# Moving the feed-forward weight loads to ScalarE's DMA queue, splitting the tile-load wait by tensor, and dropping the filler matmuls of the first three tiles

## What is computed

```python
# recurrence, per batch and head, over t
m_new = maximum(f_t + m, i_t)
C = exp(f_t + m - m_new) * C + exp(i_t - m_new) * outer(v_t, k_t)
n = exp(f_t + m - m_new) * n + exp(i_t - m_new) * k_t
y_t = sigmoid(o_t) * (C @ q_t) / maximum(abs(n . q_t), 1)
# x: (3072, 320) = y as tokens
g = maximum(x @ w_in, 0) ** 2          # w_in 320 x 2048
x2 = g @ w_out                         # w_out 2048 x 320
e = argmax(x2 @ w_gate); p = softmax(x2 @ w_gate)[e]
out = p * (maximum(x2 @ w1[e], 0) @ w2[e])   # 8 experts, 1024 wide
```

## Time and profile before

| what | before |
|---|---|
| median of three runs | 846.07 us (844.88 to 847.69) |
| the profiled execution, its own time | 849.91 us |
| its span | 848.0 us |
| PE busy | 798.2 us (94%) |
| DVE busy | 565.3 us (67%) |
| POOL busy | 378.6 us (45%) |
| ACT busy | 243.4 us (29%) |

### The profile page before, as it was taken

One profiled execution on the slowest core, in us unless ns is written; L12 is line 12 of the kernel. 1 busy time (PEld: TensorE's weight loads), 2 busy tenths in 40 slices (PEclk: granted clock), 3 DMA queues, 4 the chain that ended last, 5 costly groups with the idle time before them and its releaser, 6 DMA issues.

```text
span 848.0 us, 17409 instructions
## 1 busy us (share of the span) xinstructions
PE 798.2 (94%) x5334; PEld 759.0 (90%) x5335; DVE 565.3 (67%) x1075; ACT 243.4 (29%) x578; POOL 378.6 (45%) x346
## 2 busy tenths in 40 slices
PE   7769899999999999999999999988879999999994
PEld 7769899999999999999999999987769988898984
DVE  5758886667666767766766767465846657766662
ACT  2114334333333333333334333334000112021320
POOL 3326654533533533433434432777200263438792
PEclk9759899999999999999999999999989999999997
DMA  9955333233331442331432300545421061616640
GB/s 182 188 120 127 65 55 59 57 57 57 84 58 21 99 65 43 81 64 29 100 62 40 82 1 4 191 144 165 138 65 37 19 198 31 182 28 187 187 142 23
DMA packets 153815, 74.98 MB, mean 88 GB/s; under 512 B 107951, under 2 KB 147887, under 8 KB 153744
## 3 DMA queue, kind: packets, MB, share of 16 engines
q1 hardware_dynamic: 141552, 48.07, 27.6%
q10 hardware_dynamic: 9120, 17.30, 7.0%
q0 software_dynamic: 3072, 8.68, 2.7%
HBM read 62.89 MB, written 12.39 MB: 89 GB/s over the span
## 4 chain that ended last, share of the span: by engine, by line
PE 61%; issue 18%; POOL 7%; DVE 4%; POOLq 3%; ACT 2%; DMA 2%; SPq 2%; DVEq 0%; ACTq 0%
PE bank_h L1213 20%; PE bank_o L1377 18%; POOL expert_w L547 5%; PE bank_b L1275 5%; PE bank_o L1457 2%; PE bank_c L1280 2%; PE bank_c L1267 2%; PE bank_a L1286 2%; PE bank_h L1432 1%; PE bank_h L1359 1%; PE bank_a L1255 1%; POOLq L630 1%; PE bank_b L1255 1%; DVE decay L967 1%; PE bank_c L1294 1%
## 5 line engine op out<-in xcount | busy, mean ns | idle before, releaser
L598 POOL TENSOR_TENSOR g_lo<-g,g_hi 128x384 fp32r<-128x384 f32 x128 | 138.5, 1083 | 241.3 <-ACT g_hi L678 240.7
L547 POOL TENSOR_TENSOR expert_w<-raw,expert_w 128x1024 fp32r<-128x1024 f32 (+2 forms) x48 | 105.4, 2222 | 95.3 <-ACT expert_w L649 93.5
L678 ACT CAST g_hi<-g 128x384 fp32r<-128x384 f32 x128 | 66.0, 516 | 270.9 <-DVE g L838 262.9
L1377 PE MATMUL bank_o<-wout_hi,g_hi 128*128 128x320 f32 x384 | 129.9, 338 | 6.4 <-POOL g_lo L598 6.1
L1377 PE MATMUL bank_o<-wout_hi,g_lo 128*128 128x320 f32 x384 | 120.3, 313 | 0.0
L1377 PE MATMUL bank_o<-wout_lo,g_hi 128*128 128x320 f32 x384 | 120.1, 313 | 0.0
L1457 PE MATMUL bank_o<-expert_w,hT_hi 128*128 (+1 forms) x448 | 103.9, 320 | 6.8 <-DVE hT_lo L1156 4.5
L838 DVE TENSOR_TENSOR g<-relu 128x384 f32<-128x384 f32 x128 | 82.1, 642 | 33.8 <-ACT relu L738 19.7
L649 ACT CAST expert_w<-raw 128x1024 fp32r<-128x1024 f32 (+2 forms) x48 | 44.0, 981 | 197.1 <-PE bank_h L1436 126.3
L1377 PEld LDWEIGHTS bank_o<-wout_hi,g_hi 128*128 128x128 f32 x384 | 73.5, 191 | 11.1 <-POOL g_lo L598 7.9
L1457 PEld LDWEIGHTS bank_o<-expert_w,hT_hi 128*128 128x128 f32 x448 | 76.2, 193 | 7.9 <-issue 7.9
(11 more groups left out here) (261 smaller groups left out, 1632.4 us busy)
## 6 DMA issues: line engine op xcount, KB each, us to landing
forget_bc<-forget_rows SPq DMA_DIRECT2D x48, 256.0 KB, 4.5
raw<-in_moe_w_dram ACTq DMA_DIRECT2D x12, 512.0 KB, 3.6
raw<-in_moe_w_dram ACTq DMA_DIRECT2D x12, 480.0 KB
ex_x<-regions SPq DMA_DIRECT2D x28, 192.0 KB
q_in<-in_q_dram SPq DMA_DIRECT2D x24, 160.0 KB, 3.2
k_in<-in_k_dram SPq DMA_DIRECT2D x24, 160.0 KB, 3.9
v_in<-in_v_dram SPq DMA_DIRECT2D x24, 160.0 KB, 4.3
o_in<-in_o_gate_dram SPq DMA_DIRECT2D x24, 160.0 KB, 4.2
```

Of the source, the lines that this page charges most:

```text
L547: pool.tensor_tensor(lo, raw[0:rows, slot, 0:cols], hi[0:rows].bitcast(F32), ALU.subtract).then_inc(lo_split, 1)
L598: pool.tensor_tensor(g_lo[:, r, :], g[:, s, :], g_hi[:, r, :].bitcast(F32), ALU.subtract).then_inc(glo_ready, 1)
L678: act.copy(g_hi[:, r, :], g[:, s, :]).then_inc(ghi_ready, 1)
L1377: ins = pe.matmul(bank_o[j][:, 0:DM], part[:, r, t], w[:, f, :], start=(f == 0 and n == 0), stop=(f == NF - 1 and n == 2))
```

## The change

1. `load_ffn` moves from SP's program to ACT's. ACT issues pieces 0 to 2 right after its two exponentials of the gate rows, and after it has split the high part of piece n it issues piece n + 3. The wait on `lo_split` that guards the slot moves along.
2. `load_tile` no longer waits for all readers of the old buffers ahead of its first DMA. It issues v, q, k, o in this order, each behind a wait for that tensor's own reader: `vw_ready`, `qT_ready`, `kw_ready` with `kT_ready`, `oexp_ready`.
3. `keep_busy` runs 12 times at the start instead of 26, and not at all inside tiles 0, 1 and 2.

```diff
@@ load_tile (SP)
-                need(sp, kT_ready, n - 1)
-                need(sp, vw_ready, n - 1)
-                need(sp, kw_ready, n - 1)
-                need(sp, oexp_ready, n - 1)
-                for dst, src in ((q_in[:, par, :, 0:D], q), (k_in[:, par, :, 0:D], k), (v_in[:, par, :, 0:D], v), (o_in[:, par, :, :], o_gate)):
+                for dst, src, read in ((v_in[:, par, :, 0:D], v, vw_ready), (q_in[:, par, :, 0:D], q, qT_ready),
+                                       (k_in[:, par, :, 0:D], k, kw_ready), (o_in[:, par, :, :], o_gate, oexp_ready)):
+                    need(sp, read, n - 1)
+                    if read is kw_ready:
+                        need(sp, kT_ready, n - 1)
@@ SP's program
-            for n in range(FIRST_PIECES):
-                load_ffn(n)
             load_tile(0, 2)
             load_tile(0, 3)
-            for n in range(FIRST_PIECES, 2 * FIRST_PIECES):
-                load_ffn(n)
...
             load_tile(0, 4)
-            for n in range(2 * FIRST_PIECES, NFP - 2):
-                load_ffn(n)
             load_tile(0, 5)
-            for n in range(NFP - 2, NFP):
-                load_ffn(n)
@@ ACT's program, behind the exponentials of the gate rows
+            def load_ffn(n):
+                slot = ffn_slot(n)
+                need(act, lo_split, n + 1 - FFN_RING)
...
+            for n in range(FIRST_PIECES - 1):
+                load_ffn(n)
@@ half (ACT)
                         split_hi(ffn_slot(n), *ffn_piece(n), 32 * (n // FFN_RING + 1))
+                        if n + FIRST_PIECES - 1 < NFP:
+                            load_ffn(n + FIRST_PIECES - 1)
@@ PE's program
-            keep_busy(bank_c, 26)
+            keep_busy(bank_c, 12)
@@ mix (PE)
-                if static(b) and c < TB and d in (2, 3):
-                    keep_busy(bank_o[1], 5)
```

More of the change, by code:

```diff
@@ L390, in _ @@
             sp.dma_start(i_row[:, :], i_gate.rearrange("b h s -> (b h) s")).then_inc(gates_in, 16)
[L392 to L399, removed]
             load_tile(0, 0)
@@ L654, in _ @@
             act.activation(in_row[:, :], in_row[:, :], ACT.Exp).then_inc(gate_act, 1)
+            def load_ffn(n):
+                slot = ffn_slot(n)
+                need(act, lo_split, n + 1 - FFN_RING)
+                is_out, of = ffn_order[n]
+                if is_out:
+                    load_raw_chunks(act, slot, w_out, *cuts(NF)[of])
+                else:
+                    load_raw(act, slot, w_in, of[0], slice(of[1] * PC, (of[1] + 1) * PC))
+            for n in range(FIRST_PIECES - 1):
+                load_ffn(n)
             def start_tile(b, c):
```

## The result

| what | before | after |
|---|---|---|
| median, nine runs each on one chip | 846.12 us (844.88 to 850.91) | 853.42 us (849.69 to 854.93) |
| ratio after to before | | 1.0073, 95% interval 1.0052 to 1.0094 |
| the profiled execution, its own time | 849.91 us | 852.42 us |
| its span | 848.0 us | 850.4 us |
| its mean granted PE clock | 0.960 | 0.952 |

The change makes the kernel 0.7% slower, 6.2 us by the ratio (4.4 to 8.0). The forecast was 846.6 and its range ended at 850.0, so both were too low. Two gaps have to be explained: 2.5 us between the two profiled executions, and 7.3 us between the medians.

A forecast was written before the change was run, and what follows sets the result against it. PE, busy 798.2 of 848.0 us, was taken as the bound, so only the start could change. Terms summed to +0.51: 849.91 to 850.4 profiled, 3.8 lower for the median, 846.6; range 842.6 to 850.0.

The forecast's parts named there:

- Weights in front of the forget factors: Start: ACT's weight pieces 0 to 2 delay the forget store and read-back, +3.9 us, from 0 to 5.7.
- The split over the two hops: Forget store and read-back under equal queue time: +1.5 us on the store, +1.9 on the read-back, 3.4 together.
- weights starve both hops: Rival at the start: forget store and read-back each lose 4.4 us, 8.8 in all; +5.4, 851.5; chance 0.18.
- +1.81: Tile 1's d 3 without fillers: priced at 1.2 GHz, 5.06 us in place of 3.25.
- The median of the runs shown is 846.07, 3.8 lower; the difference is the same.: Whole kernel: the 850.4 us forecast for the profiled execution becomes 846.6 for the median.
- -1.83: Filler group at 45.85, ahead of tile 2's d 3: removing it gives back 1.83 of its 2.13 us.
- tile 2 was at this clock already: 0: Tile 2's d 3: already at 1.2 GHz before, so removing fillers costs 0.
- ACT's new instructions: ACT's program, start and block 0: issuing the weight DMAs there costs 0.
- The tile-2 wait: PE's 2.16 us wait until tile 2 landed at 30.70: earlier load removes it, -2.16.
- the store lands at 13 to 17: Sign at the start: the forget store lands at 13 to 17 in place of 12.2.
- scan near 20.5: Sign at the start: DVE's first decay scan starts near 20.5; wrong if before 18 or after 22.5.
- d 3 of tiles 0 to 2 at 3.3 us: Sign on PE: d 3 groups of tiles 0 to 2 take 3.3 us each at clock 0.50.

The follow-up runs named there:

- the repeat: The changed kernel again, unchanged, against the kernel before on another chip: ratio 1.0053 (1.0033 to 1.0073).

## Why the forecast was too low

**The term that decides was mis-sized.** The step is "Weights in front of the forget factors: +3.9, from 0 to 5.7". Its mechanism and its upper bound were right; the value inside was wrong. The slip measured 5.67, what the bound gave: all of the weights' own 1.57 MB at the rate of the read-back stage. I took the middle between equal sharing of time (3.4) and what tile 2's q had lost (4.4). Equal sharing is what failed: from 10 to 14 SP's queue had 0.3 of the packet time, and ACT's had issued its first DMA 1.2 us ahead of the store, since ACT did not wait to be free at 8.83 as I had let it. The Trainium skill ("DMA: Bandwidth & Descriptors", section "Queues, rings and completion order") has the engines take turns between queues, a whole packet at a time, which pointed to the upper end and +2.3; the measured 5.67 agrees with that direction. Turns of one packet for one packet, as the profile counts them, are not what the rows show: it was four of SP's for one of ACT's. Whether the rule or the head start made the difference isn't shown: no run had equal starts with equal packets. That 277 GB/s hit the slip exactly is partly luck, since the last 2 us before the landing carried 0.07 MB.

**The split over the two hops was wrong, their sum was bounded rightly.** I had 1.5 on the store and 1.9 on the read-back. The store took all of it (+5.66), the read-back nothing (-0.10). When the weights wait for the store, the read-back takes +2.70 instead (in both such profiles). The rival "weights starve both hops" needed 8.8 and did not come: with early weights, which are through by 18, nothing is left for the second hop to lose, as the argument against it said.

**Against the profiled execution the rest nearly held.** With all weights out of the way, the sum without this term is -3.39, so the first product should be at 56.35; it was at 57.19. With 5.67 in place of 3.9 the sum is +2.28. The chain showed +1.49. The differences can be named: tile 1's d 3 stayed mostly at 2.4 GHz, so +1.81 did not come (in the other profile of this kernel it did, and the chain showed +3.10); tile 0's slow d 3 cost 0.97 in place of 0.57; tile 2's cost 0.36 in place of 0; and 0.26 are left from steps that I had counted as unmoved, `den` at +0.52 and the transposes of q and k at -0.26 (2.28 - 1.81 + 0.40 + 0.36 + 0.26 = 1.49). The span's +2.4 holds this 1.49 only by chance, as the `ranks` copies show: it depends on where later stretches at 1.2 GHz fell.

**The second failed step is the translation to the median.** "The median of the runs shown is 846.07, 3.8 lower; the difference is the same." It isn't. With 5.67 in its place the sum would still have given only 848.4. The rest of the sum, -3.39, was measured alone in the timed runs, with the weights behind both hops: -0.8 us (-2.8 to +1.3), so at least 0.6 of the counted gain, and about 2.6, is not there in them. The likely reason is that the 3.8 are not a constant offset of profiling; the profiled execution had a mean clock of 0.960, and on other chips this kernel ran at up to 0.978. The terms -1.83 and "tile 2 was at this clock already: 0" were read from rows in which the fillers had failed. In other runs of before they mostly don't, as at 55.40 above, and by their clock that may be nearly half of them; then the change takes away a start that is 4 us shorter. The changed kernel's profiled execution lies 1.0 below its median, before's 3.8 above: that is 4.8 of the 7.3 us between the medians, and 2.5 are left between the profiles. The mis-sized term (1.8) and the gain that didn't come (2.6) bring the forecast of +0.5 to +4.9, inside the interval of the repeat (2.8 to 6.2) and of the result (4.4 to 8.0).

That the gain didn't come is measured; its reason, the clock, is supported by the runs, not settled by them: with the fillers taken out alone the kernel is as quick as before (1.0013), so the 4 us of before's better course are not lost in every run without fillers. The clocks of before's timed runs beside the result are not known either. The 6.2 and 4.5 us that the ratios of the two chips give (0.73% and 0.53%) and the scan's 5.5 agree within the intervals, about 1.7 us each way; what share of the rest is clock stays open.

**Point by point.** ACT's new instructions cost nothing that the rows show: in block 0 PE's and POOL's waits for ACT are no longer than before (the largest, POOL's `g_lo` for `g_hi`, 19.1 us in all against 20.8), and `xT_hi` of tile 2 starts at 59.87, when PE's transposes for it end (58.95 + 0.89). The tile-2 wait went. Of the marks for being right, "the store lands at 13 to 17" failed (17.97), and so did "scan near 20.5" (22.23, just inside the bound of 22.5 that I had set for being wrong). The first product came at 61.23 in place of 60.2. "d 3 of tiles 0 to 2 at 3.3 us" was right in kind for tiles 0 and 2 (1.2 GHz, 3.65 and 3.63) and failed for tile 1 (2.19). "From 140 on nothing but a shift" failed too: the distance went from -0.34 at 135 to +2.20 at 400 and +2.4 at the end.

## What to carry to other kernels

Before a bulk load goes to a queue of its own, look for a short chain of dependent transfers (a store, a wait, a read-back) that is issued in the same microseconds: with the weights issued behind it on the same queue the chain kept its 3.0 and 3.8 us here, with the weights on a second queue it did not. Put the bulk load behind a wait for that chain's landing, which gave the loss back here and no gain (0.9991), and check what travels next to it then. Where PE's clock is marginal, compare the profiled execution's time and mean clock with the timed runs first; if it lies several us off, a sum made from its rows is a sum for that course alone. And look for the same milestone in later blocks: a difference at the start can be gone 75 us later.

## What the runs showed of the hardware

- A 96 KB store that lands in 3.0 us behind its own queue's tile loads took 4.3 us with 0.52 MB and 7.2 to 8.8 us with 1.57 MB of another queue's weights in flight. While both queues had work, from 10 to 14, its queue had 0.3 of the packet time and moved four packets, mostly tile loads of some 160 bytes, for each of the weights'. I had expected half of the time.
- ACT issues DMAs while its own activation runs: the first weights were issued at 8.10, the activation ended at 8.93. Their first packets moved between 10.0 and 10.3.
- One kernel on one chip varies by 4 to 5 us along with its mean granted clock (842.0 us at 0.969 or more, 846.5 below 0.963), and twelve fillers in each of three pauses of the kernel before kept it at 0.973 or more in all 12 runs, for 0.4%. From the first product to the `ranks` copy of block 0, profiles of all versions differ by 1.9 us, with the granted clock at 0.93 to 0.95 or at 0.98 to 1.00. A kernel at 0.955 without fillers was as quick as before at 0.96 to 0.976, so the mean clock compares runs of one kernel, not kernels.
